# A linear-attention and two-stage expert kernel: the first head pair's own-token term on TensorE, another order of TensorE's steps per pair, and a longer row sum on VectorE

## The reference

```python
def _attn_ref(r, k, v, w, u):            # 4 batches, 8 heads, 768 tokens, head size 48
    state = np.zeros((B, H, D, D))
    for t in range(S):
        cur = np.einsum('bhd,bhe->bhde', u[None] * kt, vt)
        y[:, :, t] = np.einsum('bhd,bhde->bhe', rt, state + cur)
        state = wt[:, :, :, None] * state + np.einsum('bhd,bhe->bhde', kt, vt)
```

## Time and profile before

| | us |
|---|---|
| median of 3 runs | 725.61 |
| lowest and highest | 725.41 and 727.49 |
| the profiled execution, whole | 727.49 |
| its span in the profile | 725.7 |
| TensorE busy in the span | 696.0 |
| VectorE busy | 404.0 |
| GpSimd busy | 164.4 |
| first mix_state of pair 0 | 27.49 |
| mix_state of pair 1, of pair 13 | 37.64, 146.74 |

### The profile page before, as it was taken

How to read it: one execution, slowest core, us unless ns; L and a number is a source line. 1 busy time by engine, 2 the same in 40 slices (tenths; PEclk the granted TensorE clock), 3 DMA queues, 4 the chain that set the end, 5 groups by cost and what they waited for, 6 DMA issues and landing times.

```text
span 725.7 us, 12836 instructions
## 1 busy us (share of the span) xinstructions
PE 696.0 (96%) x4802; PEld 624.7 (86%) x4802; DVE 404.0 (56%) x588; ACT 279.0 (38%) x593; POOL 164.4 (23%) x156
## 2 busy tenths in 40 slices
PE   7899999996999999999999999999999999999995
PEld 6788888885899999999999988988988988889875
DVE  7799999996766665555455445234233243242331
ACT  3455555673666655545345432012022021120110
POOL 7677587822522200000000000110200200101102
PEclk9999999996999999999999999999999999999999
DMA  8987778711866554343343300000000100100001
GB/s 173 212 174 160 158 163 171 195 42 45 251 199 188 170 174 140 101 130 110 89 128 106 110 1 0 23 23 0 34 12 0 44 1 4 40 1 22 23 1 43
DMA packets 147784, 66.44 MB, mean 92 GB/s; under 512 B 118536, under 2 KB 145424, under 8 KB 147728
## 3 DMA queue, kind: packets, MB, share of 16 engines
q1 hardware_dynamic: 131696, 51.43, 28.0%
q0 software_dynamic: 3072, 9.54, 4.2%
q10 hardware_dynamic: 12960, 4.73, 2.4%
HBM read 56.14 MB, written 9.54 MB: 91 GB/s over the span
## 4 chain that ended last, share of the span: by engine, by line
PE 85%; issue 5%; DVE 4%; POOL 3%; ACT 1%; DMA 1%; SPq 0%; ACTq 0%; DVEq 0%; POOLq 0%
PE bank L1465 13%; PE bank L1466 13%; PE bank L1467 13%; PE score_banks L1465 7%; PE score_banks L1466 7%; PE score_banks L1467 7%; PE turn_banks L1466 3%; PE turn_banks L1465 3%; PE turn_banks L1467 3%; PE score_banks L1512 3%; PE turn_banks L1499 2%; PE bank L1565 2%; PE bank L1579 1%; PE bank L1554 1%; PE turn_banks L1673 1%
## 5 line engine op out<-in xcount | busy, mean ns | idle before, releaser
L691 POOL DMA_INDIRECT out_dram<-o_put,slot_tok x24 | 25.2, 1052 | 438.5 <-DVE o_put L1435 438.5
L1465 PE MATMUL bank<-hh,w2h 128*128 128x432 f32 x192 | 69.3, 361 | 0.0
L1466 PE MATMUL bank<-hl,w2h 128*128 128x432 f32 x192 | 69.0, 359 | 0.0
L1467 PE MATMUL bank<-hh,w2l 128*128 128x432 f32 x192 | 69.0, 359 | 0.0
L1386 DVE SCALAR_TENSOR_TENSOR hl<-score_banks,hh 128x432 fp32r<-128x432 f32 x48 | 29.2, 607 | 66.6 <-ACT hh L905 65.6
L956 ACT CAST gh<-g 128x512 fp32r<-128x512 f32 x36 | 22.3, 620 | 105.7 <-PE bank L1467 59.7
L1465 PE MATMUL score_banks<-xh,w1h 128*128 128x432 f32 x144 | 52.9, 367 | 0.3 <-DVE xl L1348 0.3
L905 ACT ACTIVATE hh<-score_banks 128x432 fp32r<-128x432 f32 x48 | 25.5, 531 | 70.1 <-PE score_banks L1467 70.1
L1467 PE MATMUL score_banks<-xh,w1l 128*128 128x432 f32 x144 | 51.7, 359 | 0.0
L1466 PE MATMUL score_banks<-xl,w1h 128*128 128x432 f32 x144 | 51.6, 358 | 0.0
L1465 PE MATMUL bank<-moh,gh 128*128 128x384 f32 x144 | 48.5, 337 | 0.9 <-DVE gl L1453 0.9
(11 more groups left out here) (233 smaller groups left out, 1761.9 us busy)
## 6 DMA issues: line engine op xcount, KB each, us to landing
w_raw<-in_moe_w_dram SPq DMA_DIRECT2D x77, 384.0 KB, 3.1
raw_w<-in_w_dram SPq DMA_DIRECT2D x32, 144.0 KB, 3.0
raw_k<-in_k_dram SPq DMA_DIRECT2D x32, 144.0 KB, 3.4
raw_r<-in_r_dram SPq DMA_DIRECT2D x32, 144.0 KB, 3.5
vals<-in_v_dram SPq DMA_DIRECT2D x32, 144.0 KB, 2.9
x_tokens<-x_rows ACTq DMA_DIRECT2D x32, 144.0 KB, 3.2
w_raw<-in_moe_w_out_dram SPq DMA_DIRECT2D x3, 384.0 KB, 3.2
w_more<-in_moe_w_dram SPq DMA_DIRECT2D x2, 384.0 KB
```

Source lines behind the costliest of these rows:

```text
L691: pool.indirect_dma_start(out=out, out_offset=bass.IndirectOffsetOnAxis(ap=slot_tok[:, n:n + 1], axis=0), in_=o_put[:, n % SB, :], in_offs ...
L1465: pe.matmul(dst, sh, mh_, start=first, stop=False)
L1466: pe.matmul(dst, sh, ml_, start=False, stop=False)
L1467: return pe.matmul(dst, sl_, mh_, start=False, stop=last)
```

## The change

- **Own term of pair 0.** GpSimd no longer writes it on the score diagonal. The score tile of pair 0 is cleared instead (a memset), masks of pair 0 wait for that, and own_values() multiplies v of pair 0 with the own sums into a new tile own_v. TensorE adds it in mix_values(0, h) by six matmuls of own_v with the identity per half, behind a wait for own_ready. Other pairs keep the diagonal.
- **Own sums of all pairs.** The GpSimd addition of the two halves (L612) is gone; VectorE's reduction reads 48 values per sum and not 24 (576 elements per partition and not 288).
- **GpSimd's start.** The first prefix floor comes first, own_products(0) waits for prefix_of(0), the clearing of to_rows stands behind the other clears, u_row and own_v are cleared too. own_of(0) and own_of(1) move on VectorE into the loop's first round.
- **TensorE's order.** The fills of 14, 14 and 18 matmuls go, ten stay. keys(0) and turn k of pair 1 move behind scores(0, 0). In the loop, the order ahead of scores(n, 1) becomes rows_of(n-1, 0), keys(n), turn k of pair n+1.
- **Loads.** u comes behind v of pair 0 instead of ahead of w of pair 1, into rows of 64 of which 48 are filled, so in pieces of 192 bytes instead of 1536, and waits for the cleared tile.
- **Embeddings.** tau and the embeddings share one semaphore, so that the first square waits for both; one VectorE instruction of the normalisation becomes two.

The diff, cut to its core:

```diff
-    START_WARM, LIST_WARM, TILE_WARM = 30, 24, 6
-    FILL = (10, 14, 14, 18)
+    START_WARM, NEXT_WARM, LIST_WARM, TILE_WARM = 30, 10, 24, 6
...
-    u_row = sb("u_row", [P, H, D])
+    u_row = sb("u_row", [P, H, 64])
...
-            sp.dma_start(u_row[:, :, :].rearrange("q h d -> q (h d)"),
-                         u.rearrange("(o h) d -> o (h d)", o=1).broadcast_to([P, H * D])).then_inc(u_in, 16)
             load_w(1)
             load(1, "k", k)
             load_v(0)
+            sp.wait_ge(cleared_u, 1)
+            sp.dma_start(u_row[:, :, 0:D], u.rearrange("(o h) d -> o h d", o=1).broadcast_to([P, H, D])
+                         ).then_inc(u_in, 16)
             load(1, "r", r)
             load_w(2)
...
-            pool.memset(to_rows[:, :, :, :].rearrange("q x p e -> q (x p e)"), 0.0).then_inc(rows_clear, 1)
+            pool.memset(u_row[:, :, :], 0.0).then_inc(cleared_u, 1)
             pool.memset(vals[:, :, :, :, D:].rearrange("q n c i d -> q (n c i) d"), 0.0).then_inc(zeroed, 1)
+            pool.memset(own_v[:, :, :, D:].rearrange("q c i d -> q (c i) d"), 0.0).then_inc(zeroed, 1)
             pool.memset(state[:, :, :, :].rearrange("q n c d -> q (n c d)"), 0.0).then_inc(zeroed, 1)
...
+            pool.memset(to_rows[:, :, :, :].rearrange("q x p e -> q (x p e)"), 0.0).then_inc(rows_clear, 1)
...
             def own_times_u(n):
                 p = n % PAIRS
                 both = rku[:, n % 2].rearrange("q (c h) d -> q c h d", h=2)
-                after(pool.tensor_tensor(out=both, in0=both,
-                                         in1=u_row[:, 2 * p:2 * p + 2, :].unsqueeze(1).broadcast_to([P, CH, 2, D]),
-                                         op=ALU.mult))
-                pool.tensor_tensor(out=rku[:, n % 2, :, 0:D // 2], in0=rku[:, n % 2, :, 0:D // 2],
-                                   in1=rku[:, n % 2, :, D // 2:], op=ALU.add).then_inc(own_prod, 1)
+                pool.tensor_tensor(out=both, in0=both,
+                                   in1=u_row[:, 2 * p:2 * p + 2, 0:D].unsqueeze(1).broadcast_to([P, CH, 2, D]),
+                                   op=ALU.mult).then_inc(own_prod, 1)
+
+            def own_values():
+
+                pool.wait_ge(own_sum, 1)
+                pool.wait_ge(v_in[0], 32)
+                pool.tensor_tensor(out=own_v[:, :, :, 0:D], in0=vals[:, 0, :, :, 0:D],
+                                   in1=own[:, 0].unsqueeze(3).broadcast_to([P, CH, 2, D]), op=ALU.mult
+                                   ).then_inc(own_ready, 1)
...
+            first_prefixes(0)
+            pool.memset(score[:, 0].rearrange("q c i t -> q (c i t)"), 0.0).then_inc(score_clear, 1)
             pool.wait_ge(pads, 3)
+            pool.wait_ge(prefix_ok, 1)
             own_products(0)
-            first_prefixes(0)
+            first_prefixes(1)
             pool.wait_ge(u_in, 16)
             own_times_u(0)
-            own_diagonal(0)
-            first_prefixes(1)
             own_products(1)
             own_times_u(1)
+            own_values()
             pool.wait_ge(prefix_ok, 2)
             own_diagonal(1)
-            own_products(2)
-            first_prefixes(2)
-            own_times_u(2)
-            for n in range(1, ALL - 1):
-                if n > 1:
+            for n in range(ALL - 1):
+                if n:
                     first_prefixes(n + 1)
                 if n + 2 < ALL:
                     own_products(n + 2)
                     own_times_u(n + 2)
-                pool.wait_ge(prefix_ok, n + 2)
-                own_diagonal(n + 1)
-                if n % PAIRS == 0:
+                if n:
+                    pool.wait_ge(prefix_ok, n + 2)
+                    own_diagonal(n + 1)
+                if n and n % PAIRS == 0:
                     dots_of(n // PAIRS - 1)
...
+            act.dma_start(emb_in[:, :], emb).then_inc(small_in, 16)
+            act.dma_start(tau_col[:, :], tau.rearrange("(a b) -> a b", a=1).broadcast_to([P, 1])).then_inc(small_in, 16)
             act.wait_ge(warm_ok, 1)
             act.activation(squares[:, 0:1], ones[0:E, 0:1], ACT.Sqrt).then_inc(act_seq, 1)
-            act.wait_ge(emb_in_ok, 16)
+            act.wait_ge(small_in, 32)
...
-                after(dve.scalar_tensor_tensor(out=emb_s[:, 5:6], in0=emb_s[:, 3:4], scalar=emb_s[:, 0:1],
-                                               in1=emb_s[:, 2:3], op0=ALU.mult, op1=ALU.add))
+                after(dve.tensor_tensor(emb_s[:, 4:5], emb_s[:, 3:4], emb_s[:, 0:1], ALU.mult))
+                after(dve.tensor_tensor(emb_s[:, 5:6], emb_s[:, 4:5], emb_s[:, 2:3], ALU.add))
                 after(dve.tensor_scalar(emb_s[:, 6:7], emb_s[:, 5:6], 0.5, 1e-6, ALU.mult, ALU.add))
-                dve.wait_ge(tau_in, 16)
                 after(dve.tensor_scalar(emb_s[:, 8:9], emb_s[:, 6:7], tau_col[0:E, 0:1], None, ALU.mult))
...
-                dve.tensor_reduce(out=own[:, n % 2].rearrange("q c h -> q (c h)"), in_=rku[:, n % 2, :, 0:D // 2], axis=AX, op=ALU.add
+                dve.tensor_reduce(out=own[:, n % 2].rearrange("q c h -> q (c h)"), in_=rku[:, n % 2], axis=AX, op=ALU.add
                                   ).then_inc(own_sum, 1)
...
-                dve.wait_ge(own_ready, n + 1)
+                if n:
+                    dve.wait_ge(own_ready, n + 1)
+                else:
+                    dve.wait_ge(score_clear, 1)
...
             suffix_of(0)
             keys_of(0)
             prefix_of(0)
-            own_of(0)
             receptance_of(0)
             suffix_of(1)
...
-                if n + 1 < ALL:
+                if n == 0:
+                    own_of(0)
+                elif n + 1 < ALL:
                     own_of(n + 1)
                 mask(n, 1)
                 if n + 1 < ALL:
                     prefix_of(n + 1)
                 else:
                     low_chunk(0, 2)
+                if n == 0:
+                    own_of(1)
                 carry(n)
                 if n + 1 < ALL:
...
+                if n == 0:
+                    pe.wait_ge(own_ready, 1)
+                    for c in range(HALF):
+                        for i in range(2):
+                            pe.matmul(y_of(h, i, c), own_v[:, HALF * h + c, i], ident[:, :], start=False, stop=False)
...
             turn_raw(0, "w")
-            fill(FILL[0])
+            for _ in range(NEXT_WARM):
+                pe.matmul(bank[7][:, 0:P], ones[:, :], ones[:, :], start=True, stop=True)
             turn_raw(0, "k")
             turn_raw(0, "r")
             embeddings()
-            fill(FILL[1])
             turn_raw(1, "w")
-            keys(0)
-            turn_raw(1, "k")
-            fill(FILL[2])
             scores(0, 0)
-            fill(FILL[3])
             for n in range(ALL):
-                if n and n + 1 < ALL:
+                if n:
+                    rows_of(n - 1, 0)
+                keys(n)
+                if n + 1 < ALL:
                     turn_raw(n + 1, "k")
-                if n:
-                    keys(n)
-                    rows_of(n - 1, 0)
                 scores(n, 1)
                 if n + 2 < ALL:
```

More of the change, by code:

```diff
@@ L214, in linear_attention_moe_max_mlp @@
     w_more = sb("w_more", [P, EARLY - WRAW, KD * 2 * P])
+    own_v = nc.alloc_sbuf_tensor_at("own_v", [P, CH, 2, 64], F32, offset=more_at)
+    assert 4 * CH * 2 * 64 <= cursor[0] - more_at
     assert cursor[0] <= nc.sbuf_usable_end, (cursor[0], attention_end, nc.sbuf_usable_end)
@@ L248, in sem @@
             return ctx.enter_context(nc.semaphore(name))
-        consts = sem("consts")
+        consts, cleared_u = sem("consts"), sem("cleared_u")
         pool_seq, dve_seq, act_seq = sem("pool_seq"), sem("dve_seq"), sem("act_seq")
-        emb_in_ok, tau_in, u_in, warm_ok = sem("emb_in_ok"), sem("tau_in"), sem("u_in"), sem("warm_ok")
+        small_in, u_in, warm_ok = sem("small_in"), sem("u_in"), sem("warm_ok")
         raw_in = {name: [sem(f"raw_{name}_in{i}") for i in range(RING)] for name in "wkr"}
@@ L266, in linear_attention_moe_max_mlp @@
             sem("dots_ok"), sem("dots_stored"), sem("plain_hot"), sem("plain_first"))
-        earlier_ok, fore_ok = sem("earlier_ok"), sem("fore_ok")
+        earlier_ok, fore_ok, score_clear = sem("earlier_ok"), sem("fore_ok"), sem("score_clear")
         placed, parted, apart = sem("placed"), sem("parted"), sem("apart")
@@ L780, in high_chunk @@
                              raw_chunk(s, c).rearrange("q (c f) -> q c f", c=2)).then_inc(wh_ok, 1)
-            act.dma_start(emb_in[:, :], emb).then_inc(emb_in_ok, 16)
-            act.dma_start(tau_col[:, :], tau.rearrange("(a b) -> a b", a=1).broadcast_to([P, 1])).then_inc(tau_in, 16)
+            act.dma_start(emb_in[:, :], emb).then_inc(small_in, 16)
+            act.dma_start(tau_col[:, :], tau.rearrange("(a b) -> a b", a=1).broadcast_to([P, 1])).then_inc(small_in, 16)
             act.wait_ge(warm_ok, 1)
             act.activation(squares[:, 0:1], ones[0:E, 0:1], ACT.Sqrt).then_inc(act_seq, 1)
```

(16 more changed lines are left out.)

## The result

The changed kernel takes 729.88 us (median of 4 runs, 729.72 to 729.94), the kernel before 725.51 beside it (4 runs). The ratio is 1.0055, with a 95% interval of 1.0036 to 1.0074: it is slower, by 4.4 us, and by more than the 0.3% that can be told from no change.

What follows compares the result with a forecast made beforehand. Neither TensorE nor VectorE alone but the loop through both bounds the attention: lead −2.2, pairs 2 to 13 +3.8 and +0.2, pair 14 +0.7, pair 15 −0.7; unrounded +1.7 on median 725.61 gives 727.3 us, range 724.4 to 730.0.

Steps and rivals of the forecast that it cites:

- the cold start: Rival, start: without fills TensorE idles 3.5 us, clock falls, pair 0 steps double; lead gone, 729.4 us; chance 0.2.
- the likeliest case: The forecast of 727.3 us with range 725.6 to 728.8, given chance 0.6.
- The round: Attention loop, mix_state to next mix_state: 9.41 us a pair against 9.09 before, +0.32.
- Turn k's detour: TensorE loop: rows and keys go first, so turn k ends 3.95 us after mix_state; VectorE, ready at 3.30, waits 0.65.
- VectorE's part behind it: Loop, after turn k: 5.00 us from keys to carried state with the longer sum, then 0.46 to mix_state.
- Pairs 2 to 13: 12 × 0.32 = +3.8: Attention loop: each of twelve pairs takes 0.32 us longer than the profile's 9.09, +3.8 us together.
- the start: Up to pairs 0 and 1: mix_state(0) at 25.7 instead of 27.49, pair 1 at 35.4 instead of 37.64, lead 2.2 us.
- tau's 1.1: Embeddings: the first square waits for tau, landing at 4.55 us; it went at 3.47 before, so +1.1.
- the score clear holds the prefix scan: Start, pair 0: GpSimd's memset delays VectorE's prefix scan from 10.4 to about 10.9 us; if not held, −0.5.
- own_v waits out a scan: Start: own_v on GpSimd waits for pair 1's prefix scan on VectorE, running 22.1 to 23.5 us.
- Order free: Rival, loop: VectorE is ready later than 3.30, hiding the 0.65; round 8.9, −4 to −5, 721 us; chance 0.1.
- in between: Rival, loop: the detour costs half as much, round 9.25, total 725 us; chance 0.1.

## Why the prediction was right, and where it was not

**The forecast** was 727.3 (724.4 to 730.0) with "within 0.3%" the likeliest. The time is 729.88: inside the range, at its edge, and slower by 0.6%. That it lies inside is in part luck: the upper end stood there for the cold start, and the likeliest case alone (725.6 to 728.8) misses it. The mechanism forecast is the one that runs; one term of the sum was mis-sized.

**The round: right.** Turn k's detour was put at 3.95 to keys_of; it is 3.95. VectorE's part behind it was put at 5.46; it is 5.51. The round was put at 9.41; it is 9.46. VectorE was ready at 3.44 and not 3.30, so that its wait is 0.51 and not 0.65; as turn k's end sets the round, that changed nothing. The row sum was put at 0.74; it is 0.743. The prefix scans are at 1.77. keys(15) has lost its wait. The two exchanges of TensorE's order (9.46 to 8.92 and to 8.8) show that the round follows turn k. Not foreseen: turn w waits 0.33 for keys_of, where the working had TensorE losing nothing. TensorE's own path from there (68.53 to 72.93) reaches mix_state together with VectorE's, so which of the two sets the 9.46 stays open; both start at turn k's end.

**The base of the round: the step that failed.** It is the term "Pairs 2 to 13: 12 × 0.32 = +3.8". The working took 9.09 a pair from the profile, worked out a shift of +1.7 against that execution, and put the shift on the median, 725.61. But the execution was 1.9 above that median, and the text said so without asking why: it held four pairs (3 to 6) where the addition went ahead of the scan. The typical round is 8.93 (the kernel before, run again), and 12 × 0.16 = 1.9 us are missing from "+3.8". Against its own base the sum nearly stands: +1.7 forecast for the profiled execution, +2.3 measured (729.77 − 727.49). There the start gave 0.35 more than forecast, and pairs 2 to 13 took 5.0 longer and not 4.0, by 0.05 a round and by find_experts (0.6 and not 0.2); pairs 14 and 15 came as forecast (+0.7, −0.7). Like against like, span against span of the usual execution, it is 728.0 − 723.6 = 4.4, the difference of the medians. The mean of 2.00 for the prefix scans was read as a fixed cost; it was a toss-up, of which the trace held a rarer outcome.

**The start: 1.1 better at pair 0, 0.35 at pair 1.** Right were the scan at 7.5 (7.59) and tau's 1.1 (1.25 of waiting, 4.62 against 3.47). Wrong was that the score clear holds the prefix scan: 1.38 us of memset and an undisturbed scan of 1.77 stand beside each other, so the end of the bracket that I did not take was the true one, worth 0.5. Wrong too was that own_v waits out a scan: it took 1.15 from 19.99, ahead of the prefix scan at 20.39. It won because keys_of(1) was late. With the fills, where keys_of(1) is 0.9 earlier, the scan goes first and own_v takes 2.6 (from 18.79 in the version with turn k first and tau); mix_state(0) comes no sooner. The pair between them then takes 9.3 to 9.4 us (forecast: 9.66) and not 10.48, and so the lead at pair 1 was only 0.35 better than forecast. One reading of a row was off, without effect on the sum: the turn in the earlier trace rows takes 0.81; the 0.87 there is mix_state.

By the Trainium skill (SBUF — State Buffer, "SBUF: two separate sides"), a VectorE operation with two SBUF inputs contends only with a GpSimd operation that reads SBUF, and whoever starts first keeps the ports for its whole instruction. The trace agrees with both: 1.77 beside the memset of 1.38, and 2.37 = 0.60 + 1.77 for the addition.

**The cold start: its mechanism was there, its price elsewhere.** The clock did fall and was back before own_v, as argued against that rival; it cost pair 0 nothing. It cost keys_of(1) 0.94 us, which the working had "in VectorE's shade", and through that it let own_v go ahead of the scan, which is what costs pair 1 its 0.9 to 1.0: two traces without fills and at the low clock, where the scan still came first, do not pay it. In the trace of the changed kernel with fills the gain is lost again with the late gather.

**Order free, and in between: fell.** The waits of 0.5 us are there and are paid; the round is 9.46, not 8.9 or 9.25.

**The ledger**, from medians: order −6.1 when undone, tau −1.2, the long sum a gain of 0.2 to 1.2. The start's lead (2.4 us at pair 1 with turn k first, against before, run again) is 2.1 from the long sum and 0.3 from all the rest, in which tau costs 0.7 to 1.2; so the own term of pair 0 on TensorE, GpSimd's new order, the loads and the missing fills bring 1.0 to 1.5 together. No run undoes the own term, GpSimd's order or the loads alone, so what the own term itself is worth is not shown.

## What to carry to other kernels

When two engines hand work back and forth in a loop, neither's busy share bounds it: add up the loop through both, and put first, on the engine that feeds, what the other waits for. Before a shift is put on a median, ask why the profiled execution differs from it; where two operations contend and start within 0.15 us of each other, as here, their order can be a toss-up, and a mean over one trace is not the kernel's. A gain in one stage is seen in the time only if the next stage's transfers still come in time, so read the marks of every stage behind it.

## What the runs showed of the hardware

- GpSimd's addition and VectorE's scan exclude each other, and the order changes from run to run of one program: 0.80 and 2.27, or 2.37 and 1.77. In the kernel before, without the addition, 11 times lie within 0.8 us; with it, 24 lie within 2.5.
- The same between own_v (1.15) and the prefix scan in the start: 0.95 us at pair 1, in nine traces always one of two values.
- A memset of 128x1536 on GpSimd (1.38) leaves a VectorE scan at 1.77; beside an affine_select of the same size it took 1.83.
- One packet of instruction code (0.02 MB, 1.2 us of one DMA engine) beside the third gather went with 1.3 to 1.4 us of waiting on TensorE, in two traces of two, and with 0.7 to 1.0 us on the rest of the program. With 24 matmuls more ahead it came earlier, and the wait was 0.30. That the packet is the cause is not shown.
